# Block means of the values: from transposed sums on VectorE instead of twelve matmuls per head

## The chip, the core and the metric

One NeuronCore of a Trainium2 chip runs the whole program. Its engines each take their own instructions strictly in the order written: TensorE (PE) multiplies, VectorE (DVE) and ScalarE (ACT) work elementwise and reduce, GpSimd (POOL) does the same more slowly, and SyncE (SP) issues transfers between HBM and the core's memory. Engines meet through semaphores: an instruction may wait until a counter has reached a value, and everything behind it on its engine waits with it. The metric is the device time of one execution in microseconds.

## The reference

Attention with a window of 16 keys to either side of the query's own, plus one summary key and value per block of 32 keys, and behind it two layers of experts that this change leaves alone. With B = 4 batch elements, H = 8 heads, S = 768, D = 64:

```python
block, window = (32, 16)
nb = S // block                                     # 24
k_sum = k.reshape(B, H, nb, block, D).max(axis=3)
v_sum = v.reshape(B, H, nb, block, D).mean(axis=3)  # the block means of the values
scores_l = scale * np.matmul(q, k.transpose(0, 1, 3, 2))      # kept where |i - j| < window
scores_s = scale * np.einsum('bhsd,bhnd->bhsn', q, k_sum) + np.log(block)
a = softmax(concat([masked scores_l, scores_s]))
out = np.matmul(a, np.concatenate([v, v_sum], axis=2))
```

`v_sum` is what the change computes in another way.

## The kernel before

**Tiling.** The attention stage handles two heads at a time, a "pair": 4 batch elements of 4 pairs make 16 pairs, counted here by m = 0 to 15. A pair has PU = 3 units of 256 queries. A unit is: scores (L670, 16 matmuls, queries against a 96-key span and 24 block maxima), maxima on VectorE (L1231, L1234), exponentials on ScalarE (L998), a transpose (L679, copied out at L1006), the product with the values (L707, counted by the semaphore `pv_done`), the division on VectorE (L1240 to L1247, `x_done`), and a transpose of the result (L721).

**Steps.** All engines run the same software pipeline, written out by hand. In step n, TensorE does scores of unit n, the transpose of unit n-2, `values` of unit n-3 and `transpose_rows` of unit n-4. VectorE does `maxima` of unit n and `normalise` of unit n-3. ScalarE does the exponentials of unit n. `block_maxima` (the key summary) runs on VectorE in the steps with n % 3 of 0 and 1. Steps 0 to 5 are a prologue; a loop of 12 steps per batch element follows. The router's logits (L730, TensorE) and `route_shift` and `route` (VectorE) run in steps 14 to 17 of each group of 12, that is, in the steps 2 to 5 of the batch element that follows.

**Block means.** The values arrive as `va[m % 4]`, a tile with 96 keys on the partitions, for 12 overlapping windows of 64 queries, from the input `v_win` (585 KB per pair). `means` (L682 to L691) multiplies 12 slices of this tile by a constant matrix `average`, and accumulates them in a part of a PSUM bank, in step n = 3(m-1)+1 for pair m. `take_means` (L1198) copies the 24x128 result out in the same step, and GpSimd's `spread_means` (L528) writes it below the values, where L707 reads it. GpSimd builds `average` once at the start (L531 to L538).

**Transfers.** SyncE's queue loads keys and values. In its loop over batch elements, for each pair position hp (here G = 4b + hp, counted through), it waits for `spans_done` and issues the key load for the pair four later, then waits for `pv_done` of the last unit of pair G (reached in step 3G+5) and issues the value load for the pair four later. Since it is in order, the key load of position G is issued right behind the value load of position G-1. On the last batch element there is neither. At hp = 1 of a later batch element it also stores the last columns of `x` (L436). ScalarE's queue loads the queries (L980) in steps with n % 3 = 2 and stores `x` (L984) in steps with n % 3 = 0.

Of the kernel before, what the change touches and what calls it, by code (L numbers as in the profile page):

```python
# [10 lines left out]
ALU = mybir.AluOpType  # L11
ACT = mybir.ActivationFunctionType
AXX = mybir.AxisListType.X


P = 128
B, H, S, D = 4, 8, 768, 64
# [94 lines left out]

def two_layers_of_experts(nc, queries, k, v_win, modality_id, w_gate, modality_bias, w1, w2,
                          w_gate2, w1b, w2b, out):
    ctx = ExitStack()
    with ctx:
# [127 lines left out]
        k_loaded = [sem(f"k_loaded{i}") for i in range(HP)]  # L244
        vw_loaded = [sem(f"vw_loaded{i}") for i in range(HP)]
        pads_ready = sem("pads_ready")
        mask_ready = sem("mask_ready")
# [41 lines left out]
        span_mask = sa("span_mask", [P, PW])  # L289
        average = sa("average", [WK, NQ, NB])  # L290
        vst = [sa(f"vst{i}", [PW, 2, D]) for i in range(2)]
# [110 lines left out]
        def _(sp):  # L402
            def load_k(b, hp):
                sp.dma_start(kraw[hp][:, :, WINDOW:WINDOW + S], k[bass.ds(b, 1), hp, :, :, :].rearrange("o d h s -> (o d) h s")
                             ).then_inc(k_loaded[hp], 16)

            def load_v(b, hp):
                sp.dma_start(va[hp][0:WK, :, :, :], v_win[bass.ds(b, 1), hp, :, :, :, :].rearrange("o p h j w -> (o p) h j w")
                             ).then_inc(vw_loaded[hp], 16)

            load_k(0, 0)
            load_k(0, 1)
            load_v(0, 0)
            sp.dma_start(wg[:, :, :], w_gate.rearrange("(c p) e -> p c e", p=P)).then_inc(small_loaded, 16)
            sp.dma_start(bias2[:, :, :], bass.AP(modality_bias.tensor, 0, [[0, P], [E, 2], [1, E]])).then_inc(small_loaded, 16)
# [4 lines left out]
            with sp.Fori(0, B) as b:  # L420
                for hp in range(HP):
# [4 lines left out]
                    def refill_v(nb, nhp):  # L426
                        sp.wait_ge(pv_done, UNITS * b + PU * (hp + 1))
                        load_v(nb, nhp)

                    with sp.If(b < B - 1):  # L430
                        nb = nc.s_assert_within(b + 1, 0, B - 1, skip_runtime_bounds_check_because="b < B - 1 here")
                        refill_k(nb, hp)
                        refill_v(nb, hp)
# [54 lines left out]
        def _(pool):  # L488
# [35 lines left out]
            def spread_means(m):  # L524
                pool.wait_ge(means_taken, m + 1)
                if m >= HP:
# [3 lines left out]

            avg = average[:, :, :]  # L531
            pick = lambda pattern, base, per: chain(g.affine_select(out=avg, in_=avg, compare_op=ALU.is_ge, fill=0.0, base=base,
                                                                    pattern=pattern, channel_multiplier=per))
            chain(g.memset(avg, 1.0 / BLOCK))
            pick([[QB, NQ], [-BLOCK, NB]], -WINDOW, 1)
            pick([[-QB, NQ], [BLOCK, NB]], WINDOW + BLOCK - 1, -1)
            pick([[-2, NQ], [1, NB]], 0, 0)
            pick([[2, NQ], [-1, NB]], 1, 0)  # L538
            for t in va:
# [114 lines left out]
        def _(pe):  # L654
# [27 lines left out]
            def means(b, m, n):  # L682
                pe.wait_ge(vw_loaded[m % HP], 16 * (b + m // HP + 1))
                if m or not isinstance(b, int):
                    pe.wait_ge(means_taken, HP * b + m)
                if n >= 5:
                    pe.wait_ge(x_done, UNITS * b + n - 4)
                for j in range(NQ):
                    last = mm(bank[4 + (n + 1) % 2][WK:PW, MEAN0:MEAN0 + 2 * D], average[:, j, :], va[m % HP][0:WK, :, j, 0:D],  # L689
                              start=j == 0, stop=j == NQ - 1)  # L690
                last.then_inc(means_made, 1)  # L691

            def values(b, n):

                hp, i = n // PU, n % PU
                if i == 0:
                    pe.wait_ge(vsum_done, HP * b + hp + 1)
                pe.wait_ge(pt_out, UNITS * b + n + 1)
# [467 lines left out]
        def _(dve):  # L1166
# [12 lines left out]
            def block_maxima(b, m, h):  # L1179
# [6 lines left out]
                vec.tensor_reduce(ksum[:, h, :], own_keys, AXX, ALU.max).then_inc(bmax_done, 1)  # L1186

            def first_spans():
                dve.wait_ge(pads_ready, 1)
# [8 lines left out]
            def take_means(b, m, n):  # L1198
                dve.wait_ge(means_made, HP * b + m + 1)
                if n >= 3:  # L1200
                    dve.wait_ge(pv_done, UNITS * b + n - 2)
                if m >= 2:
                    dve.wait_ge(vsum_done, HP * b + m - 1)
                vec.tensor_copy(vst[m % 2][WK:PW, :, :].rearrange("p h d -> p (h d)"), bank[4 + (n + 1) % 2][WK:PW, MEAN0:MEAN0 + 2 * D]
                                ).then_inc(means_taken, 1)

            mask_rows(kbt[0])
            block_maxima(0, 0, 0)
            block_maxima(0, 0, 1)
            first_spans()  # L1210
            mask_rows(kbt[1])
            per = 10

# [37 lines left out]
            def unit(b, n, own):  # L1251
# [9 lines left out]
                if n % PU < 2:  # L1261
                    own(block_maxima, PU * m, m, n % PU)
                if n == 4:
                    token_biases()
# [454 lines left out]
def laid_out(inputs):  # L1719
# [10 lines left out]
    rows[..., :D] = _np.where(outside[:, :, None], 0, v[:, :, :, key, :]).transpose(0, 1, 4, 2, 3, 5)  # L1730
    laid["v_win"] = rows
    laid["moe2_w_gate"] = _np.asarray(inputs["moe2_w_gate"]).T
    return laid


_INS = ['q', 'k', 'v_win', 'moe_modality_id', 'moe_w_gate', 'moe_modality_bias', 'moe_w1', 'moe_w2',
        'moe2_w_gate', 'moe2_w1', 'moe2_w2']
# [19 lines left out]
```

## Time and profile before

| | us |
|---|---|
| median of 3 runs | 1066.01 (1064.84 to 1074.94) |
| the profiled execution | 1066.68, its span 1064.9 |
| attention stage | 0 to about 217 of the span |
| TensorE busy over the span | 898.2 (84%) |
| VectorE busy over the span | 681.6 (64%) |
| GpSimd busy over the span | 285.1 (27%) |
| `v_win` loads | 16 of 585 KB, median 6.4 us to landing |
| `k` loads | 16 of 384 KB, median 9.1 us to landing |

A granted clock of 1.00 stands for TensorE's 2.4 GHz, 0.50 for 1.2 GHz. The chain that ended last goes 27% through L777 and 11% through L898, which are the expert layers. Within the first 240 us it goes 17.0% through L689 (`means`), 14.0% through L670, 9.1% through L730, 8.9% through L707, 8.2% through L679.

### The profile page before, as it was taken

How to read it: one execution, taken by the hardware profiler on the slowest of the kernel's cores; microseconds unless marked ns; L12 is line 12 of the kernel's file. 1: busy time of each engine (PE TensorE's matmuls, PEld its weight loads, DVE VectorE, ACT ScalarE, POOL GpSimd, SP SyncE). 2: the span in 40 equal slices, each digit the busy share in tenths (PEclk: the TensorE clock that was granted, in tenths of full speed). 3: DMA queues.
4: the chain of work that ended last, by engine and by line, in shares of the span. 5: the costliest groups of instructions: out<-in, count | busy, mean ns of one | idle time of the engine just before them, and what ended most of it. 6: DMA issues, size and time to landing. Idle time of an engine off the chain costs nothing.

```text
span 1064.9 us, 21948 instructions
## 1 busy us (share of the span) xinstructions
PE 898.2 (84%) x7342; PEld 733.7 (69%) x7343; DVE 681.6 (64%) x1998; ACT 305.5 (29%) x626; POOL 285.1 (27%) x390
## 2 busy tenths in 40 slices
PE   4899999915899999999996233999898989998995
PEld 3787878714688888888885122868686867687884
DVE  5757576575666666666665567777777768674440
ACT  2544454505322212222221003223232322223330
POOL 5733344101012111111220005050515151414501
PEclk9999999956899999999998655999999999999998
DMA  9676675915011111111110123414141414155100
GB/s 195 122 160 135 133 153 100 280 50 185 11 51 40 50 40 40 40 40 40 40 50 20 24 71 119 159 51 169 50 169 54 165 61 159 61 204 172 32 29 30
DMA packets 45631, 99.94 MB, mean 94 GB/s; under 512 B 6736, under 2 KB 19072, under 8 KB 45440
## 3 DMA queue, kind: packets, MB, share of 16 engines
q1 hardware_dynamic: 26816, 61.63, 19.8%
q0 software_dynamic: 8064, 26.46, 7.9%
q10 hardware_dynamic: 10688, 11.01, 4.9%
q8 instruction: 39, 0.64, 0.2%
q14 instruction: 24, 0.20, 0.1%
HBM read 79.57 MB, written 19.51 MB: 93 GB/s over the span
## 4 chain that ended last, share of the span: by engine, by line
PE 69%; DVE 18%; issue 4%; POOL 3%; ACT 2%; DMA 2%; DVEq 0%; ACTq 0%; SPq 0%; POOLq 0%
PE bank L777 27%; PE bank L898 11%; PE bank L912 9%; PE bank L689 4%; PE bank L670 3%; PE bank L848 3%; DVE w_low L1649 2%; PE bank L730 2%; PE bank L707 2%; PE bank L801 2%; PE bank L679 2%; POOL slot_hot L635 2%; DVE xl L1653 1%; DVE ge L1517 1%; ACT xh L1042 1%
## 5 line engine op out<-in xcount | busy, mean ns | idle before, releaser
L1404 DVE SCALAR_TENSOR_TENSOR bank<-y,wg 128x512 f32<-128x512 f32 x200 | 132.0, 723 | 2.9
L635 POOL TENSOR_SCALAR slot_hot<-iota_l,mlo 128x128 bf16<-128x128 f32 x96 | 72.0, 766 | 214.7 <-DVE mlo L1622 214.7
L898 PE MATMUL bank<-xh,w_high 128*128 128x384 f32 x256 | 94.3, 368 | 16.1 <-DVE hl L1639 8.9
L777 PE MATMUL bank<-w_high,hh 128*128 x200 | 83.2, 416 | 13.2 <-DVE hl L1393 13.2
L777 PE MATMUL bank<-w_high,xh 128*128 x200 | 82.7, 414 | 10.7 <-DVE gates L1386 10.7
L592 POOL DMA_INDIRECT y_rows<-y,sidx x25 | 25.0, 998 | 243.2 <-DVE bank L1404 243.2
L898 PE MATMUL bank<-xh,w_low 128*128 128x384 f32 x256 | 88.1, 344 | 0.0
L898 PE MATMUL bank<-xl,w_high 128*128 128x384 f32 x256 | 87.9, 344 | 0.0
L1042 ACT ACTIVATE hh<-bank 128x512 fp32r<-128x512 f32 x50 | 27.1, 595 | 203.1 <-PE bank L801 203.1
L1418 DVE TENSOR_SCALAR y<-bank,gates 128x512 f32<-128x512 f32 x25 | 18.8, 751 | 101.1 <-PE bank L777 101.1
L912 PE MATMUL bank<-w_high,hh 128*128 128x512 f32 x192 | 82.3, 429 | 0.0
L1042 ACT ACTIVATE w_high<-w_landed 128x1024 fp32r<-128x1024 f32 x64 | 63.1, 1049 | 66.0 <-DMA w_landed<-in_moe_w 66.0
L777 PE MATMUL bank<-w_low,hh 128*128 x200 | 80.5, 403 | 0.0
L777 PE MATMUL bank<-w_high,hl 128*128 x200 | 80.3, 402 | 0.0
L777 PE MATMUL bank<-w_low,xh 128*128 x200 | 80.3, 402 | 0.0
L777 PE MATMUL bank<-w_high,xl 128*128 x200 | 80.2, 401 | 0.0
L1649 DVE TENSOR_TENSOR w_low<-w_landed,w_high 128x1024 fp32r<-128x1024 f32 x64 | 77.8, 1219 | 0.8
L848 PE MATMUL bank<-ge,cb 128*8 128x16 bf16 x1344 | 42.3, 170 | 41.7 <-DVE ge L1517 41.6
L912 PE MATMUL bank<-w_high,hl 128*128 128x512 f32 x192 | 75.7, 394 | 0.0
L912 PE MATMUL bank<-w_low,hh 128*128 128x512 f32 x192 | 75.5, 393 | 0.0
L848 PEld LDWEIGHTS bank<-ge,cb 128*8 128x8 bf16 x1344 | 36.2, 83 | 54.6 <-DVE ge L1517 50.8
L1118 ACT ACTIVATE hh<-bank 128x384 fp32r<-128x384 f32 x64 | 31.5, 492 | 140.2 <-PE bank L898 140.2
(285 smaller groups left out, 1932.5 us busy)
## 6 DMA issues: line engine op xcount, KB each, us to landing
w_landed<-in_moe_w SPq DMA_DIRECT2D x16, 2048.0 KB, 10.5
va<-in_v_win SPq DMA_DIRECT2D x16, 585.0 KB, 6.4
raw_w<-in_moe_w SPq DMA_DIRECT2D x4, 2048.0 KB, 11.3
k_raw<-in_k SPq DMA_DIRECT2D x16, 384.0 KB, 9.1
q_eye<-in_q ACTq DMA_DIRECT2D x16, 384.0 KB, 7.4
x_rows<-x ACTq DMA_DIRECT2D x12, 384.0 KB, 10.2
wg<-in_moe_w_gate SPq DMA_DIRECT2D x1, 2048.0 KB, 25.8
x_rows<-x SPq DMA_DIRECT2D x4, 387.0 KB, 7.2
```

The source lines that it names most:

```text
L592: pool.indirect_dma_start(out=dst[:, :], out_offset=bass.IndirectOffsetOnAxis(ap=sidx[:, 0:1], axis=0), in_=y[:, 0:w], in_offset=None).the ...
L635: last = g.tensor_scalar(slot_hot[:, j, :], iota_l[:, :], mlo[:, j:j + 1], None, ALU.is_equal)
L670: last = mm(bank[n % 2][QB * s_:QB * s_ + QB, PW * (2 * t + h):PW * (2 * t + h) + PW], qe[hp % 2][:, h, QB * j:QB * j + QB], kbt[hp % 2][: ...
L689: last = mm(bank[4 + (n + 1) % 2][WK:PW, MEAN0:MEAN0 + 2 * D], average[:, j, :], va[m % HP][0:WK, :, j, 0:D], start=j == 0, stop=j == NQ - 1)
L777: last = mm(ps, lhs[a][:, c, :], rhs[b](c), start=c == 0 and t == 0, stop=c == n - 1 and t == 2)
L848: last = mm(bank[7][0:E, 0:KSEARCH], cb[:, j, :], ge[:, j, :], start=j == 0, stop=j == TC - 1)
L898: last = mm(bank[fc % 2][:, 0:CAP], w[:, q % 2, c, f], a[:, c, :], start=c == 0 and t == 0, stop=c == KC - 1 and t == 2)
L912: last = mm(bank[2 + t % 2][:, :], a[:, c, rows], w[:, q % 2, c, :], start=c == 0 and n == 0, stop=c == FC - 1 and n == 2)
L1042: copy = lambda o, a: nc.scalar.activation(o, a, ACT.Copy)
L1118: nc.scalar.activation(hh2[:, fc, :], bank[fc % 2][:, 0:CAP], ACT.Relu).then_inc(hhigh_done, 1)
L1404: stt(bank[6 + e % 2][:, :], y[:, 0:DM], 1.0, wg2[:, e, :], ALU.mult, ALU.mult, accum_out=y[:, DM + e:DM + e + 1]).then_inc(l2_out, 1)
L1649: tt(low, whole, high.bitcast(F32), ALU.subtract).then_inc(low_done, 1)
```

## The change

The host lays out a second copy of the values, `v_cols`, of shape batch, pair, 2 x 64 head channels, 768 keys. SyncE loads 384 KB of it per pair into one of two new tiles `vcols`. VectorE sums 32 keys at a time (`sum_values`, a 128x768 reduction to 128x24, into one of two tiles `vsums`), for pair m in step 3m-4. TensorE turns this with one matmul against the identity in the step where `means` stood, and `take_means` multiplies by 1/32 as it copies. The constant `average` and its five GpSimd instructions are gone. The wait for the values' arrival moves from `means` to `values`.

```diff
@@ sync
+            def load_cols(b, m):
+                sp.dma_start(vcols[m % 2][:, :], v_cols[bass.ds(b, 1), m, :, :, :].rearrange("o h d s -> (o h d) s")
+                             ).then_inc(vc_loaded[m % 2], 16)
             load_k(0, 0)
             load_k(0, 1)
             load_v(0, 0)
+            load_cols(0, 0)
+            load_cols(0, 1)
...
+                    def refill_cols(cb_, m):
+                        sp.wait_ge(vsums_made, HP * b + m - 1)
+                        load_cols(cb_, m % HP)
+
+                    if hp < HP - 2:
+                        refill_cols(b, hp + 2)
                     with sp.If(b < B - 1):
                         nb = nc.s_assert_within(b + 1, 0, B - 1, skip_runtime_bounds_check_because="b < B - 1 here")
+                        if hp >= HP - 2:
+                            refill_cols(nb, hp + 2)
                         refill_k(nb, hp)
                         refill_v(nb, hp)
@@ gpsimd
-            avg = average[:, :, :]
...
-            chain(g.memset(avg, 1.0 / BLOCK))
@@ tensor
             def means(b, m, n):
-                pe.wait_ge(vw_loaded[m % HP], 16 * (b + m // HP + 1))
+                pe.wait_ge(vsums_made, HP * b + m + 1)
...
-                for j in range(NQ):
-                    last = mm(bank[4 + (n + 1) % 2][WK:PW, MEAN0:MEAN0 + 2 * D], average[:, j, :], va[m % HP][0:WK, :, j, 0:D],
-                              start=j == 0, stop=j == NQ - 1)
-                last.then_inc(means_made, 1)
+                mm(bank[4 + (n + 1) % 2][WK:PW, MEAN0:MEAN0 + 2 * D], vsums[m % 2][:, :], ident[:, :],
+                   start=True, stop=True).then_inc(means_made, 1)
@@ vector
+            def sum_values(b, m):
+
+                dve.wait_ge(vc_loaded[m % 2], 16 * (HP // 2 * b + m // 2 + 1))
+                if m >= 2:
+                    dve.wait_ge(means_made, HP * b + m - 1)
+                vec.tensor_reduce(vsums[m % 2][:, :], vcols[m % 2][:, :].rearrange("p (n t) -> p n t", t=BLOCK), AXX, ALU.add
+                                  ).then_inc(vsums_made, 1)
...
             first_spans()
+            sum_values(0, 0)
             mask_rows(kbt[1])
+            sum_values(0, 1)
...
                 if n % PU < 2:
                     own(block_maxima, PU * m, m, n % PU)
+                else:
+                    own(sum_values, PU * (m + 1), m + 1)
```

SyncE's queue, positions G = 0 and 1 of the first batch element, before. `k_raw` and `va` are the key and value tiles; the line of an ISA row is that of a wait.

```order
L404 ISA [waits spans_done]
L404 DMA k_raw0<-in_k 64x2x768
L427 ISA
L408 ISA [waits pv_done]
L408 DMA va0<-in_v_win 96x1560
L430 UNCONDITIONAL_BRANCH
L430 COMPARE_AND_BRANCH
L423 ISA
L404 ISA [waits spans_done]
L404 DMA k_raw1<-in_k 64x2x768
```

The same place now, from the value load of position 0 to that of position 1:

```order
L411 ISA [waits pv_done]
L411 DMA va0<-in_v_win 96x1560
L445 UNCONDITIONAL_BRANCH
L440 REGISTER_ALU
L415 ISA [waits vsums_made]
L415 DMA v_cols1<-in_v_cols 128x768
L445 COMPARE_AND_BRANCH
L407 ISA [waits spans_done]
L407 DMA k_raw1<-in_k 64x2x768
L436 ISA
L411 ISA [waits pv_done]
L411 DMA va1<-in_v_win 96x1560
```

The load of `v_cols` of position 1 (it is for pair 3) stands behind the wait for `pv_done` of position 0 and behind its value load, and ahead of the key load.

VectorE, the end of step 4 and step 5, before (`mbias` is the last of the token biases; then maxima of unit 5, division of unit 2, and the loop begins with step 6):

```order
L1223 TENSOR_TENSOR mbias<-mbias,mtmp 128x192 [waits dve_chain]
L1231 TENSOR_REDUCE nmax1<-bank1 128x4 [waits exp_done,scores_done,dve_chain]
L1234 TENSOR_SCALAR nmax1<-nmax1 128x4 [waits max_done]
L1240 TENSOR_SCALAR rtmp<-bank4 128x4 [waits pv_done]
L1242 RECIPROCAL rinv<-rtmp 128x4 [waits sums_read]
L1247 TENSOR_TENSOR x<-bank4,rinv 128x2x128 [waits inverted]
```

The same place now:

```order
L1241 TENSOR_TENSOR mbias<-mbias,mtmp 128x192 [waits dve_chain]
L1249 TENSOR_REDUCE nmax1<-bank1 128x4 [waits exp_done,scores_done,dve_chain]
L1252 TENSOR_SCALAR nmax1<-nmax1 128x4 [waits max_done]
L1258 TENSOR_SCALAR rtmp<-bank4 128x4 [waits pv_done]
L1260 RECIPROCAL rinv<-rtmp 128x4 [waits sums_read]
L1265 TENSOR_TENSOR x<-bank4,rinv 128x2x128 [waits inverted]
L1201 TENSOR_REDUCE v_sums1<-v_cols1 128x24 [waits means_made,vc_loaded1]
```

The sum of pair 3 stands at the end of step 5, ahead of all of step 6. The rows of the wait for `pv_done` are the same.

TensorE, step 7, before (scores of unit 7, transpose of unit 5, `means` of pair 3, `values` of unit 4):

```order
L670 MATMUL bank1<-k_bias0,q_eye0 64x120 x7
L679 MATMUL bank3<-ident,probs2 120x128 [waits pt_out,exp_done]
L679 MATMUL bank3<-ident,probs2 120x128 x3
L683 ISA
L689 MATMUL bank4<-va3,average 24x128 [waits x_done,means_taken,vw_loaded3]
L689 MATMUL bank4<-va3,average 24x128 x11
L707 MATMUL bank4<-va1,pt0 64x65 [waits x_done,pt_out]
```

And now:

```order
L679 MATMUL bank1<-k_bias0,q_eye0 64x120 x7
L688 MATMUL bank3<-ident,probs2 120x128 [waits pt_out,exp_done]
L688 MATMUL bank3<-ident,probs2 120x128 x3
L692 REGISTER_ALU
L697 MATMUL bank4<-ident,v_sums1 24x128 [waits x_done,means_taken,vsums_made]
L715 MATMUL bank4<-va1,pt0 64x65 [waits x_done,pt_out]
```

One matmul stands where 12 were (each f32 matmul shows twice in the trace), and it waits for VectorE's sum.

## Rows read from the trace of the kernel before

**Rows 1.** Windows of one pair and of one with logits: busy per engine, clock, DMA.

```profile
59.24:69.85 10.61, 10.43 (x139) 8.29 (x140) 7.09 (x19) 5.98 (x19) 4.78 (x7) 1.00 0.83 168
69.85:85.20 15.35, 15.35 (x187) 13.72 (x187) 8.41 (x21) 6.46 (x22) 6.17 (x8) 1.00 0.47 94
```

**Rows 2.** Groups by line and form, 0 to 240 us: count, busy us, mean ns, idle before.

```profile
L689 PE MATMUL bank<-va,average 96*24 96x128 f32 x384 | 47.4, 281 | 0.2 <-POOLq L541 0.2
...
L1186 DVE TENSOR_REDUCE ksum<-k_raw 64x24 f32<-64x768 f32 x32 | 29.8, 934 | 2.8 <-DMA k_raw<-in_k 2.8
...
L1204 DVE COPY vst<-bank 24x128 f32<-24x128 f32 x16 | 4.7, 297 | 36.0 <-PE bank L707 29.6 <-PE bank L689 6.3
```

**Rows 3.** Timeline 57 to 61 us, step 11 and the start of 12.

```profile
57.00 1.04 PE L670 MATMUL bank<-k_bias,q_eye 128*64 128x120 f32 x16
...
58.55 0.69 PE L707 MATMUL bank<-va,pt 120*64 120x65 f32 x16
...
58.74 0.64 DVE L1231 TENSOR_REDUCE nmax<-bank 128x4 f32<-128x480 f32 x1
...
59.43 0.33 SPq L408 DMA_DIRECT2D va<-in_v_win  x1
...
59.92 0.36 ACT L998 ACTIVATE probs<-bank,nmax 128x120 f32<-128x120 f32 x1
59.94 0.42 DVE L1247 TENSOR_TENSOR x<-bank,rinv 128x256 f32<-128x256 f32 x1
...
60.16 0.55 SPq L404 DMA_DIRECT2D k_raw<-in_k  x1
60.17 0.87 ACT L998 ACTIVATE probs<-bank,nmax 128x120 f32<-128x120 f32 x3
```

**Rows 4.** Timeline of SyncE's queue: first and last value load, and one with a store.

```profile
35.84 0.34 SPq L408 DMA_DIRECT2D va<-in_v_win  x1
...
96.15 0.33 SPq L408 DMA_DIRECT2D va<-in_v_win  x1
...
97.63 0.57 SPq L404 DMA_DIRECT2D k_raw<-in_k  x1
...
168.50 0.33 SPq L408 DMA_DIRECT2D va<-in_v_win  x1
```

**Rows 5.** Issues with us to landing: key loads at 36.6, 49.7 (158.6 alike), 86.2, 97.6, 148.7.

```profile
k_raw<-in_k SPq DMA_DIRECT2D x1, 384.0 KB, 6.3
...
k_raw<-in_k SPq DMA_DIRECT2D x1, 384.0 KB, 10.2
...
k_raw<-in_k SPq DMA_DIRECT2D x1, 384.0 KB, 5.8
...
k_raw<-in_k SPq DMA_DIRECT2D x1, 384.0 KB, 12.0
...
k_raw<-in_k SPq DMA_DIRECT2D x1, 384.0 KB, 9.4
```

**Rows 6.** The same for the first load behind the prologue's, issued at 12.3.

```profile
k_raw<-in_k SPq DMA_DIRECT2D x1, 384.0 KB, 15.6
```

**Rows 7.** Timeline of TensorE, 131 to 137 us: logits of unit 11, then step 17.

```profile
131.08 1.85 PE L730 MATMUL bank<-wg,xt 128*128 128x8 f32 x16
132.86 1.81 PE L670 MATMUL bank<-k_bias,q_eye 128*64 128x120 f32 x16
134.60 1.11 PE L679 MATMUL bank<-ident,probs 128*120 128x128 f32 x4
135.64 1.01 PE L707 MATMUL bank<-va,pt 120*64 120x65 f32 x16
```

**Rows 8.** Timeline of VectorE: the first and the last instruction of `route`, first batch element.

```profile
87.33 0.83 DVE L1278 TENSOR_TENSOR leq<-lg,lmax 128x48 f32<-128x48 f32 x1
...
90.53 0.17 DVE L1285 COPY x<-lidx 128x6 f32<-128x6 f32 x1
```

**Rows 9.** Windows again: step 17's end, and the weight prefetch after the attention's loads.

```profile
134.00:136.00 2.00, 2.00 (x18) 1.36 (x16) 1.97 (x3) 0.26 (x1) 1.76 (x2) 0.50 0.00 0
...
210.00:212.00 2.00, 2.00 (x18) 2.00 (x17) 0.00 (x0) 0.40 (x2) 0.00 (x0) 0.87 0.99 405
```

More of the change, by code:

```diff
@@ L110, in val, with two_layers_of_experts @@
     return k + x.c if x.c else k
-def two_layers_of_experts(nc, queries, k, v_win, modality_id, w_gate, modality_bias, w1, w2,
+def two_layers_of_experts(nc, queries, k, v_win, v_cols, modality_id, w_gate, modality_bias, w1, w2,
                           w_gate2, w1b, w2b, out):
@@ L245, in two_layers_of_experts @@
         vw_loaded = [sem(f"vw_loaded{i}") for i in range(HP)]
+        vc_loaded = [sem(f"vc_loaded{i}") for i in range(2)]
+        vsums_made = sem("vsums_made")
         pads_ready = sem("pads_ready")
@@ L289, in two_layers_of_experts @@
         span_mask = sa("span_mask", [P, PW])
-        average = sa("average", [WK, NQ, NB])
+        vcols = [sa(f"v_cols{i}", [P, S]) for i in range(2)]
+        vsums = [sa(f"v_sums{i}", [P, NB]) for i in range(2)]
         vst = [sa(f"vst{i}", [PW, 2, D]) for i in range(2)]
@@ L529, in spread_means @@
                 g.nop().then_inc(vsum_done, 1)
-            avg = average[:, :, :]
-            pick = lambda pattern, base, per: chain(g.affine_select(out=avg, in_=avg, compare_op=ALU.is_ge, fill=0.0, base=base,
-                                                                    pattern=pattern, channel_multiplier=per))
-            chain(g.memset(avg, 1.0 / BLOCK))
[L535 to L538, printed above, removed]
             for t in va:
@@ L696, in values @@
                 if i == 0:
+                    pe.wait_ge(vw_loaded[hp % HP], 16 * (b + hp // HP + 1))
                     pe.wait_ge(vsum_done, HP * b + hp + 1)
@@ L1203, in take_means @@
                     dve.wait_ge(vsum_done, HP * b + m - 1)
-                vec.tensor_copy(vst[m % 2][WK:PW, :, :].rearrange("p h d -> p (h d)"), bank[4 + (n + 1) % 2][WK:PW, MEAN0:MEAN0 + 2 * D]
-                                ).then_inc(means_taken, 1)
+                vec.tensor_scalar(vst[m % 2][WK:PW, :, :].rearrange("p h d -> p (h d)"), bank[4 + (n + 1) % 2][WK:PW, MEAN0:MEAN0 + 2 * D],
+                                  1.0 / BLOCK, None, ALU.mult).then_inc(means_taken, 1)
             mask_rows(kbt[0])
@@ L1731, in laid_out @@
     laid["v_win"] = rows
+    laid["v_cols"] = v.transpose(0, 1, 2, 4, 3)
     laid["moe2_w_gate"] = _np.asarray(inputs["moe2_w_gate"]).T
     return laid
-_INS = ['q', 'k', 'v_win', 'moe_modality_id', 'moe_w_gate', 'moe_modality_bias', 'moe_w1', 'moe_w2',
+_INS = ['q', 'k', 'v_win', 'v_cols', 'moe_modality_id', 'moe_w_gate', 'moe_modality_bias', 'moe_w1', 'moe_w2',
         'moe2_w_gate', 'moe2_w1', 'moe2_w2']
```

## The prediction

> **What bounds the kernel now.** I read three views. First the windows cut at SyncE's value loads, one pair of heads each [rows 1]: in a plain pair of 10.61 us TensorE is busy for 10.43, VectorE for 7.09, ScalarE for 5.98, GpSimd for 4.78. So TensorE sets the pace, and it also does where the logits come in (15.35 of 15.35). Then the groups by line [rows 2]: `means` is 47.4 us over 16 pairs, some 2.7 us of each pair, and about 5.3 in the first. What it is worth is at most that. Third the timeline of one step 11 with both queues in it [rows 3], because the change puts a new transfer into SyncE's queue and a new wait into VectorE's, and busy time says nothing of either.
>
> **What is saved.** 384 matmul records become 32. One matmul of two records is about 0.2 us, so TensorE loses 2.5 us per pair, 40 in all. GpSimd loses five short instructions at the start; they cost nothing, as VectorE will be waiting there for a transfer (below). The scaled copy in `take_means` is the same 24x128 copy of 0.30 us [rows 2].
>
> **What is added on VectorE.** Sixteen reductions of 128x768. The nearest row is the reduction of 64x768 with the same 768 elements on a partition, 0.93 us [rows 2]; I take it as it is. VectorE would be busy for 8.0 us of a pair, and TensorE for 7.9. Were there nothing else, a pair would take 8 to 9 us.
>
> **What is added as a wait, which decides.** The sum of pair m stands at the end of step 3m-4. Its transfer is issued by SyncE at position G = m-2, behind the wait for `pv_done` of position G-1. That is the `values` of unit 3G-1 = 3m-7, which TensorE executes in step 3G+2 = 3m-4. It is the same step, and VectorE's last work ahead of the sum (dividing unit 3m-7) waits for the same event. So the transfer is issued when VectorE is one division, under a microsecond, from needing it. The free buffer does not help: `vsums_made` was reached long before. SyncE is late because it is in order and waits for something else.
>
> Rows give the price. In step 11 `values` ends at 59.24 [rows 3]; call this V. SyncE issues the value load at V+0.2, and what stands next in its queue at V+0.9 (now keys, then `v_cols`, with keys behind it). VectorE has finished at V+1.1. The key load in that slot has the same 384 KB behind the same 585 KB, beside the same query load. Of the eleven such loads from 36.6 to 158.6, nine have no store of `x` on SyncE ahead of them; they land 5.8 to 10.2 us after issue, mean 8.3, the first 6.3 and the last 10.2 [rows 5]. I take 8.3. VectorE resumes at R = V+9.2.
>
> What is queued behind: on VectorE all of the next step, first the maxima, for which ScalarE's exponentials wait, then TensorE. TensorE still has step 3G+3 and the scores and transpose of 3G+4 to do, about 5 us, and then stops at the new matmul, which waits for the sum. This idle time is some 5 us per pair.
>
> From R to the next V: sum 0.93; maxima from R+1.0; the exponentials begin 1.18 after the maxima (58.74 to 59.92) and end 1.12 later (61.04) [rows 3], so R+3.3; the scores of step 3G+5, which wait for their bank, begin at R+3.5; from there to the end of `values` is 2.24 (57.00 to 59.24) [rows 3]. So V comes at R+5.8, and the period is 9.2 + 5.8 = 15.0 us instead of 10.6.
>
> **TensorE's clock.** Where it was granted 0.50, at 134 to 136 us [rows 9], the three groups on this path took 1.81, 1.11 and 1.01 us [rows 7] instead of 1.04, 0.65 and 0.69: the stretch of 2.24 becomes 3.8, and the transposes ahead of it add 0.3. A period is then 16.9. In this trace the attention stage kept 1.00 nearly throughout, but TensorE never idled 5 us in it, and the fall in [rows 9] came with no idle time, behind the logits' narrow matmuls. So the rows do not say what a stalled stretch gets, and both ends stand; I take the middle, 15.95.
>
> The Trainium skill, in "TensorE: Matmul & The Clock Gate", section "HAM oscillation — how this bites in real kernels", says that a wait for a transfer which repeats in every iteration sends the clock to half each time. By it the period would be 16.9 and the kernel some 1140 us. No row here shows it.
>
> **The sum.** Stalls come for pairs 3 to 14. (Pairs 0 and 1 are loaded at the start; on the last batch element SyncE no longer waits for `pv_done`, so pair 15 comes with pair 14.)
> - Start: pair 2's load goes into the slot of the key load issued at 12.3, which landed at 27.9 [rows 6]; with two more `v_cols` loads ahead, at some 2 us each, it lands at 32. The first V is at 37.8 instead of 35.6: +2.2.
> - Eleven periods, first to last value load, take 132.7 us now (35.84 to 168.50) [rows 4]. They become 11 x 15.95 = 175.5.
> - In two batch elements the logits of one unit, 1.7 us [rows 7], and `route`, 3.4 us from 87.33 to 90.70 [rows 8], lie between R and the next V: +10.2. The other logits and `route_shift` lie under the stall.
> - Twice a store of `x` stands ahead of the load: issued 1.48 instead of 0.73 behind the value load [rows 4], landing after 12.0 and 9.4 [rows 5] instead of 8.3: +6.3.
> - After the last stall TensorE has its earlier work done; the scores of step 41 come about 14.5 to 15 us behind V, where they now come 13.2 behind: +1.5. The last `means` saves 2.5: together -1.0.
>
> 2.2 + (175.5 + 10.2 + 6.3 - 132.7) - 1.0 = +60.5 us. Full clock throughout gives +50, half throughout +71 (with slower logits some +73). The profiled execution took 1066.7 and the median is 1066.0, so they are one number here: 1127 us, with 1116 and 1140 at the ends of the clock. With landings of 5.8 or 10.2 instead of 8.3 it would be 28 less or 21 more.
>
> **Rivals.**
> 1. *A stall at the full clock throughout*, 1116, or *at half throughout*, 1140. For the first speaks that this stage kept 1.00 through short gaps, for the second that the idle time is three or four times longer than any of them. 20% each.
> 2. *The transfer is quick.* The windows show 405 GB/s when large loads run alone [rows 9], against 168 in the attention stage [rows 1]. At 405, the 585 and 384 KB ahead and in it would take 2.4 us, and a landing of about 4 us would be possible. The eleven periods then cost 47 us less, and the kernel takes about 1080 or, at the full clock, 1069. Against it: the measured loads in this very slot. In "DMA: Bandwidth & Descriptors", section "Anatomy of one DMA — SWDGE (gpsimd) path", the Trainium skill gives 2.0 us plus the bytes at 436 GB/s, an estimate of 4.3 us for both together. The rows of this slot disagree with it by a factor of two, so I give the case 6%.
> 3. *The stall is hidden and the kernel faster.* The mechanism would be that the sum's load is in flight a step earlier, or VectorE a landing late anyway. The turning point is a landing of 3.8 us: 11 x (0.9 + 3.8 + 5.8) plus the other terms is 132.7. Fully hidden, VectorE at 8.0 us busy and TensorE at 7.9 give periods of about 9, and the kernel comes to 1066.7 - 11 x 1.6 - 5 for the slow first `means` - 5 for the last pairs = 1039. No row speaks for it; the order of SyncE's queue speaks against it. 3%.
> 4. *Contention*: the store of `x` by ScalarE now starts 2 to 3 us before the next burst rather than behind it, and takes engine time from the `v_cols` load; landings of 11 us give 1160. 8%.
>
> The forecast, a stall per pair with the clock between its levels, has 43%.
>
> **How the numbers follow.** Slower by over 1% (about what a measurement of this kernel tells from no change) holds forecast, 1, 4 and half of 2: 0.94. Within 1% is the rest of 2: 0.03. Faster is 0.03. The range drops rivals 2 and 3 and most of 4: from 1100 (full clock, landings of 6.8) to 1152 (half clock, landings of 9.3).
>
> **What would show it.** Right: VectorE idle ahead of the `v_cols` reduction with the transfer as releaser, some 8 us at a time, 12 times, about 95 in all; value loads of SyncE 15 to 17 us apart; the new matmul on TensorE waiting for VectorE; the attention stage ending near 277 instead of 217, and everything behind it unchanged. Wrong, if value loads stay below 11 us apart, if VectorE's wait is under 4 us, or if the stage's granted clock is 1.00 throughout (then 1116).

## The result, and the profile after

| | before | after |
|---|---|---|
| median, us | 1066.13 of 4 runs (1064.84 to 1074.94) | 1120.35 of 4 runs (1120.16 to 1120.9) |
| span of the profiled execution | 1064.9 | 1118.5 |
| last store of `x` by SyncE, the end of the attention stage | 217.70 | 267.37 |
| from there to the end of the span | 847.2 | 851.1 |
| first and last value load of SyncE's loop | 35.84, 168.50 | 36.96, 215.57 |

The ratio is 1.0477, 95% interval 1.044 to 1.0513: 54 us slower, where 61 were forecast. 49.7 of the 53.6 us between the spans lie in the attention stage. Ratios, here and below, go by executions in the chip's faster state alone; the profiled execution of `e2` was not in it, so only the ratio of `e2` is used.

The page of after, the busy times and the chain that ended last:

```profile
PE 893.5 (80%) x6990; PEld 722.9 (65%) x6991; DVE 683.6 (61%) x2014; ACT 305.6 (27%) x626; POOL 281.5 (25%) x385
...
PE 61%; DVE 17%; DMA 11%; issue 5%; ACT 2%; POOL 2%; SPq 1%; DVEq 0%; ACTq 0%; POOLq 0%
PE bank L785 25%; PE bank L906 11%; DMA v_cols<-in_v_cols 10%; PE bank L920 8%; PE bank L679 3%; PE bank L856 3%; DVE w_low L1669 2%; PE bank L738 2%; PE bank L715 2%; PE bank L809 2%; POOL slot_hot L644 2%; PE bank L688 1%; DVE xl L1673 1%; DVE ge L1537 1%; ACT xh L1050 1%
```

TensorE's busy time has hardly fallen (898.2 to 893.5), although 352 matmul records are gone. And the landing of `v_cols` is now a tenth of the chain. The waits, 0 to 290 us (engine, line, releaser: us in total, times, longest):

```profile
DVE v_sums L1201 <- DMA v_cols<-in_v_cols: 93.5, 15, 11.3
...
PE bank L697 <- DVE v_sums L1201: 50.6, 13, 8.4
```

The groups of the changed lines, which answer to [rows 2]:

```profile
L679 PE MATMUL bank<-k_bias,q_eye 128*64 128x120 f32 x768 | 63.3, 320 | 14.1 <-DVE k_bias L1212 10.8 <-POOLq L539 1.7 <-issue 1.3
...
L1201 DVE TENSOR_REDUCE v_sums<-v_cols 128x24 f32<-128x768 f32 x16 | 15.2, 952 | 93.5 <-DMA v_cols<-in_v_cols 93.5
...
L697 PE MATMUL bank<-ident,v_sums 128*24 128x128 f32 x32 | 8.1, 346 | 52.4 <-DVE v_sums L1201 50.6 <-DVE vst L1220 1.9
...
L1220 DVE TENSOR_SCALAR vst<-bank 24x128 f32<-24x128 f32 x16 | 4.8, 297 | 1.4 <-PE bank L715 0.7
```

47.4 us of `means` became 8.1. But the unchanged scores now take 320 ns a matmul. The kernel before took 279:

```profile
L670 PE MATMUL bank<-k_bias,q_eye 128*64 128x120 f32 x768 | 51.9, 279 | 18.8 <-DVE k_bias L1196 12.2 <-POOLq L522 4.2 <-DMA q_eye<-in_q 1.3
```

The timeline from the value load of position 1 to that of position 3, two periods (start, duration, engine, line, and in brackets the idle time before and its releaser):

```profile
51.57 0.34 SPq L415 DMA_DIRECT2D v_cols<-in_v_cols  x1
...
61.53 0.95 DVE L1201 TENSOR_REDUCE v_sums<-v_cols 128x24 f32<-128x768 f32 x1 [9.96 <-DMA v_cols<-in_v_cols]
...
62.53 0.62 PE L697 MATMUL bank<-ident,v_sums 128*24 128x128 f32 x2 [7.27 <-DVE v_sums L1201]
...
64.77 1.86 PE L679 MATMUL bank<-k_bias,q_eye 128*64 128x120 f32 x16
...
68.31 0.33 SPq L411 DMA_DIRECT2D va<-in_v_win  x1
...
69.01 0.35 SPq L415 DMA_DIRECT2D v_cols<-in_v_cols  x1
...
74.45 0.95 DVE L1201 TENSOR_REDUCE v_sums<-v_cols 128x24 f32<-128x768 f32 x1 [5.24 <-DMA v_cols<-in_v_cols]
...
81.36 0.33 SPq L411 DMA_DIRECT2D va<-in_v_win  x1
```

This is the loop of the prediction: issue, landing (9.9 and 5.4 us), VectorE stopped for it, TensorE stopped for VectorE, the path to the next value load, and with it the next issue. The windows show what each stop does to TensorE (us, busy of PE, PEld, DVE, ACT, POOL, clock, share of the transfer engines, GB/s):

```profile
56.00:60.00 4.00, 0.00 (x0) 0.00 (x0) 0.00 (x0) 0.00 (x0) 0.00 (x0) 1.00 1.03 212
60.00:64.00 4.00, 1.47 (x18) 1.07 (x18) 2.37 (x7) 0.72 (x3) 0.00 (x0) 0.55 0.30 63
64.00:68.00 4.00, 4.00 (x43) 3.05 (x40) 3.83 (x9) 2.84 (x9) 0.22 (x1) 0.60 0.37 102
68.00:72.00 4.00, 3.76 (x59) 2.91 (x56) 1.10 (x5) 2.51 (x8) 3.42 (x5) 1.00 0.66 175
...
40.00:160.00 120.00, 84.64 (x886) 66.67 (x887) 58.23 (x148) 44.63 (x137) 37.86 (x56) 0.76 0.64 140
```

For 4 us no engine works at all. When TensorE resumes, its clock is 0.55 and then 0.60 in two windows, and 1.00 in the third. The stall therefore costs twice: the idle time, and the slow stretch behind it, which stands on the path. How long that stretch lasts differs. Behind the stall that ended at 144.8 us logits followed, and the clock stood at 0.50 from 148 to 158 us, although TensorE was busy there without a break:

```profile
151.00:154.00 3.00, 3.00 (x16) 3.00 (x15) 0.70 (x3) 1.39 (x5) 2.70 (x3) 0.50 0.71 154
154.00:158.00 4.00, 4.00 (x34) 3.34 (x35) 0.00 (x0) 0.59 (x2) 1.32 (x2) 0.50 1.01 249
```

### The profile page after: what moved, and what is told of

The parts are those of the page before. It is cut to its first block, busy times and chain, and to the rows that moved or that the text cites. A ratio compares the mean times of both kernels' runs of the same rounds, so it can differ in the third digit from the quotient of the medians.

```text
span 1118.5 us, 21342 instructions
## 1 busy us (share of the span) xinstructions
PE 893.5 (80%) x6990; PEld 722.9 (65%) x6991; DVE 683.6 (61%) x2014; ACT 305.6 (27%) x626; POOL 281.5 (25%) x385
## 4 chain that ended last, share of the span: by engine, by line
PE 61%; DVE 17%; DMA 11%; issue 5%; ACT 2%; POOL 2%; SPq 1%; DVEq 0%; ACTq 0%; POOLq 0%
PE bank L785 25%; PE bank L906 11%; DMA v_cols<-in_v_cols 10%; PE bank L920 8%; PE bank L679 3%; PE bank L856 3%; DVE w_low L1669 2%; PE bank L738 2%; PE bank L715 2%; PE bank L809 2%; POOL slot_hot L644 2%; PE bank L688 1%; DVE xl L1673 1%; DVE ge L1537 1%; ACT xh L1050 1%
## 5 line engine op out<-in xcount | busy, mean ns | idle before, releaser
L785 PE MATMUL bank<-w_high,hh 128*128 x200 | 83.7, 419 | 15.0 <-DVE hl L1413 14.9
L906 PE MATMUL bank<-xh,w_low 128*128 128x384 f32 x256 | 88.2, 344 | 0.0
L1006 ACT ACTIVATE probs<-bank,nmax 128x120 f32<-128x120 f32 x192 | 53.4, 363 | 103.9 <-DVE nmax L1252 103.8
L679 PE MATMUL bank<-k_bias,q_eye 128*64 128x120 f32 x768 | 63.3, 320 | 14.1 <-DVE k_bias L1212 10.8
```

The lines of the kernel that those rows point to most:

```text
L679: last = mm(bank[n % 2][QB * s_:QB * s_ + QB, PW * (2 * t + h):PW * (2 * t + h) + PW], qe[hp % 2][:, h, QB * j:QB * j + QB], kbt[hp % 2][: ...
L785: last = mm(ps, lhs[a][:, c, :], rhs[b](c), start=c == 0 and t == 0, stop=c == n - 1 and t == 2)
L906: last = mm(bank[fc % 2][:, 0:CAP], w[:, q % 2, c, f], a[:, c, :], start=c == 0 and t == 0, stop=c == KC - 1 and t == 2)
L1006: last = nc.scalar.activation(probs[n % 3][:, a, :], bank[n % 2][:, PW * a:PW * a + PW], ACT.Exp, bias=nmax[n % 2][:, a:a + 1], scale=SCALE)
```

## The experiments

The median of before moved between the groups of runs (1066.8, 1072.2, 1069.1 and 1067.9 us), so ratios are compared. The other columns are each kernel's profiled execution: TensorE's granted clock and the busy share of the transfer engines in one window, and SyncE's last store of `x`.

| kernel | ratio to before, 95% | clock and share of transfer engines, 40 to 160 us | attention stage ends |
|---|---|---|---|
| before | 1 | 0.99, 0.73 | 217.7 |
| after | 1.0477 (1.044, 1.0513) | 0.76, 0.64 | 267.4 |
| `e1` after, load a pair earlier | 1.0005 (0.997, 1.0039) | 0.91, 0.89 | 215.3 |
| `e2` after, four buffers | 0.9964 (0.9923, 1.0004) | | |
| `e3` after, no `v_cols` reloads | 0.988 (0.9812, 0.9949) | 0.93, 0.80 | 207.3 |
| `e4` before, with the `v_cols` loads | 1.002 (0.9993, 1.0046) | 0.99, 0.91 | 216.6 |
| `e5` after, TensorE kept busy | 1.0457 (1.0365, 1.0549) | 0.94, 0.66 | 272.0 |
| `e6` after, sum a step later | 1.0454 (1.038, 1.0527) | 0.79, 0.66 | 262.3 |
| `e7` `e1` with four query buffers | 0.9972 (0.9939, 1.0004) | 0.91, 0.94 | 214.8 |
| `e8` before with four query buffers | 1.0007 (0.9976, 1.0038) | 0.99, 0.76 | 218.3 |
| `e11` `e1`, no key reloads | 0.9909 (0.9874, 0.9943) | 0.94, 0.78 | 205.6 |
| `e10` `e3`, no key reloads | 0.9735 (0.9682, 0.9787) | 0.96, 0.67 | 194.6 |
| `e12` before, change in even pairs | 0.9942 (0.9909, 0.9974) | 0.97, 0.84 | 213.7 |
| `e13` before, no key reloads | 1.0012 (0.9991, 1.0033) | 0.96, 0.53 | 220.5 |

What follows the attention stage took 846 to 855 us in these profiles, so a few microseconds of a total can come from there; the last column is free of that.

### Is it the place of the load, or its bytes?

`e1_pair_earlier`: the same loads, each one position earlier in SyncE's queue, and that of pair 2 ahead of the loop.

```diff
+            sp.wait_ge(vsums_made, 1)
+            load_cols(0, 2)
...
-                    if hp < HP - 2:
-                        refill_cols(b, hp + 2)
+                    if hp < HP - 3:
+                        refill_cols(b, hp + 3)
```

> The changed kernel, but SyncE issues the load of v_cols one pair earlier: at position G it loads pair G+3 and not G+2 (pair 2 goes ahead of the loop). Same loads, same two buffers, same waits on VectorE; only the place in SyncE's order moves. Theory (SyncE issues it in the step that needs it): a load now has a whole pair, 8 to 9 us, to land in some 7.7, so VectorE's wait falls from 93.5 us to under 15 and value loads of SyncE come 8.5 to 10 us apart; 1040 to 1055 us in all. Rival (the added traffic or VectorE's reductions cost it): the wait moves elsewhere and the time stays above 1090.

`e4_traffic`: the kernel before with the change's sixteen loads at the change's places, which nobody reads.

```diff
+                    def refill_cols(cb_, m):
+                        sp.wait_ge(vc_loaded[m % 2], 16 * (HP // 2 * b + m // 2))
+                        load_cols(cb_, m % HP)
```

> The kernel before, plus the 16 loads of v_cols at the very places in SyncE's queue where the change has them, which nobody reads; means stays with its 24 matmuls per pair. Theory: the traffic hides under TensorE, 1065 to 1075 (queries may land 1 to 2 us late in some pairs). Rival (contention of transfers is what costs the change its 54 us): above 1085.

Measured: 1068.03 us (ratio 1.0005) and 1069.24 (1.002). Moving the load alone takes all of the loss away, and the bytes alone cost nothing. So the place of the load in SyncE's order is the cause. But `e1` was expected at 1040 to 1055, and stayed level with before. The waits of `e1`, 0 to 240 us:

```profile
DVE v_sums L1203 <- DMA v_cols<-in_v_cols: 27.6, 8, 9.5
...
PE bank L681 <- DMA q_eye<-in_q: 12.5, 5, 6.3
```

VectorE's 93.5 us have shrunk to 27.6, and TensorE waits for queries, which it hardly did before. The same ten microseconds in `e1`, then in `e4`:

```profile
60.00:70.00 10.00, 4.96 (x42) 3.87 (x44) 2.64 (x7) 1.11 (x4) 3.10 (x5) 0.53 1.04 213
```

```profile
60.00:70.00 10.00, 10.00 (x131) 8.25 (x130) 6.99 (x18) 5.37 (x17) 4.17 (x7) 1.00 1.06 191
```

In both the transfer engines are full (share 1.04 and 1.06). In `e4` TensorE, with `means` still to do, is never stopped by them. In `e1` it has less to do, catches up with the loads, and stands. The timeline of `e1` shows for what:

```profile
65.05 1.87 PE L681 MATMUL bank<-k_bias,q_eye 128*64 128x120 f32 x16 [6.28 <-DMA q_eye<-in_q]
...
65.28 0.95 DVE L1203 TENSOR_REDUCE v_sums<-v_cols 128x24 f32<-128x768 f32 x1 [5.75 <-DMA v_cols<-in_v_cols]
```

Queries and `v_cols` are late together, and the scores behind the stop run at half clock (1.87 us instead of 1.04). The median landing of a query load between 40 and 160 us went from 7.5 us before to 11.0, that of a key load from 8.8 to 13.2.

The queries are issued by ScalarE and the added loads by SyncE. The Trainium skill, in "DMA: Bandwidth & Descriptors", section "Issuing engines are not separate DMA queues", says that loads of different issuers run on the same 16 engines and interleave. The trace agrees: with the added loads on SyncE's queue, the landings of ScalarE's query loads became longer too.

### More buffers

`e2_four_buffers`: four tiles for `v_cols`, loads four pairs ahead.

```diff
-        vc_loaded = [sem(f"vc_loaded{i}") for i in range(2)]
+        vc_loaded = [sem(f"vc_loaded{i}") for i in range(HP)]
...
-                        sp.wait_ge(vsums_made, HP * b + m - 1)
+                        sp.wait_ge(vsums_made, HP * b + m - 3)
...
-                        if hp >= HP - 2:
-                            refill_cols(nb, hp + 2)
+                        refill_cols(nb, hp + 4)
```

> The changed kernel with four v_cols buffers, each load issued four pairs ahead, as keys and values are; all four of the first batch element in the prologue, behind the keys and values of the same pair. Theory: no wait for v_cols in the loop at all; a pair is 8 to 9 us, set by VectorE (8.0 busy) and TensorE (7.9); 1035 to 1050, and no more than 8 us below the kernel that issues one pair earlier. Rival (transfers crowd each other): the stage is bound by landings of queries or keys, and it is no faster than the one-pair version.

`e7_four_queries`: `e1` with four tiles for the queries, loaded four pairs ahead. `e8_before_four_q`: the same tiles in the kernel before.

```diff
-                pe.wait_ge(q_loaded[hp % 2], 16 * (HP // 2 * b + hp // 2 + 1))
+                pe.wait_ge(q_loaded[hp % HP], 16 * (b + hp // HP + 1))
...
-                    m = n // PU + 2
+                    m = n // PU + HP
```

> The version that loads v_cols one pair earlier, and in addition four buffers for the queries instead of two, each loaded four pairs ahead. Theory (with the stall gone, the gain is eaten by queries that land late once pairs are shorter, and by the lower clock behind these waits): TensorE's wait for queries (12.5 us) is gone, pairs come 8.2 to 9.5 us apart, 1040 to 1052. Rival (VectorE, now as busy as TensorE, holds the pace by itself, or transfers as a whole): above 1060.

> The kernel before with the same four buffers for the queries, nothing else. Theory: queries were on time there in all but one place (1.3 us), so 1062 to 1067. Rival (late queries held the kernel before as well): under 1058.

Measured: 1065.92 (0.9964), 1068.8 (0.9972) and 1071.55 (1.0007). The first two miss what the theory of a single late load expected; for `e8` the ratio says, as expected, that queries did not hold the kernel before. In `e7` the wait for queries is gone, and the wait for `v_cols` stayed. The total between 30 and 210 us, and the longest of these waits:

```profile
DVE v_sums L1218 <- DMA v_cols<-in_v_cols: 30.1, 6, 12.8
...
36.41 0.95 DVE L1218 TENSOR_REDUCE v_sums<-v_cols 128x24 f32<-128x768 f32 x1 [12.83 <-DMA v_cols<-in_v_cols]
```

Median landings rose to 12.3 us (queries), 13.3 (`v_cols`), 14.5 (keys) and 11.5 (values, 6.0 before). Issuing earlier moved the wait from one load to another, and in `e7` 12.8 of its 30.1 us to the start, ahead of the sum of pair 2. With every landing longer, what is short is most likely transfer time. A version with four buffers for the queries and for `v_cols` together was not run.

### Taking bytes away

`e3_no_reload`: `v_cols` is loaded twice at the start, and never again. `e10_no_k_no_cols` leaves out the key loads behind the first batch element too. `e11_early_no_k` leaves these out in `e1`, and `e13_before_no_k` in the kernel before.

```diff
@@ e3
-                    if hp < HP - 2:
-                        refill_cols(b, hp + 2)
...
-                dve.wait_ge(vc_loaded[m % 2], 16 * (HP // 2 * b + m // 2 + 1))
+                dve.wait_ge(vc_loaded[m % 2], 16)
@@ e10, e11, e13
-                        refill_k(nb, hp)
...
-                    dve.wait_ge(k_loaded[m % HP], 16 * (b + m // HP + 1))
+                    dve.wait_ge(k_loaded[m % HP], 16)
```

> The changed kernel without any load of v_cols after the first two: every later pair sums the values of pair 0 or 1 again, so its block means are those of the wrong pair, and 14 loads of 384 KB are left out. It prices the change without its transfers. Theory: about 1030 to 1045, the saved matmuls minus VectorE becoming the bound; the difference to the four-buffer kernel is what the traffic costs, under 8 us. Rival (VectorE's 16 reductions are what costs): above 1060.

> The version that loads v_cols one pair earlier, without loading the keys again after the first batch element: later batch elements use the keys of the first, and 12 loads of 384 KB are left out. Theory (with v_cols the transfer engines are full at 175 to 190 GB/s and 10.6 us a pair, so TensorE's gain cannot show): with another 384 KB per pair gone, the volume is that of the kernel before, VectorE's wait for v_cols is under 10 us, and it takes 1050 to 1060, some 10 below the one-pair version. Rival (the engines' own order holds the pace): within 4 us of the one-pair version.

> The changed kernel without any load of v_cols after the first two and without loading the keys again: block means and keys of later pairs are those of earlier ones, 26 loads are left out. Theory (transfers set the pace): 1.39 MB a pair need about 8 us, as much as VectorE and TensorE; 1040 to 1050, 8 or more below the version that leaves out v_cols alone. Rival (below 1.8 MB a pair transfers no longer matter; VectorE and the chain from maxima to exponentials do): within 4 us of it.

> The kernel before without reloading the keys after the first batch element, so that the later ones use the first one's keys and the output is not the reference's. It is the control for the two kernels that gained 10 to 14 us from leaving the key loads out. Theory (in the kernel before TensorE sets the pace and the transfer engines have room, 0.81 of them busy between 40 and 80 us, so that bytes taken away buy nothing): 1065 to 1071, ratio 0.997 to 1.002. Rival (leaving the key loads out shortens any version by itself, because they delay the other loads or because VectorE or GpSimd start earlier): ratio 0.991 or less, some 10 us faster, and the gains of the other two kernels would say nothing of a second bound.

Measured: 1058.57 (0.988), 1061.38 (0.9909), 1044.88 (0.9735) and 1069.38 (1.0012). `e10` and `e13` lie in their expected ranges, `e11` 1 us above its own. `e3` missed its 1030 to 1045: without any wait for `v_cols` behind the start only 13 us were won, and its waits still show late queries:

```profile
PE bank L675 <- DMA q_eye<-in_q: 7.3, 4, 4.0
```

The four make one picture. In the changed kernel 384 KB less per pair are worth about 1% (`e11` against `e1`, `e3` against `e1`), and 768 KB less 2.7%. In the kernel before, the same key loads taken away are worth nothing (`e13`), nor do 384 KB more cost anything (`e4`). So in these kernels the bytes matter only where TensorE no longer covers them. The first two windows are of `e1` and `e10`, the last of `e13`:

```profile
40.00:80.00 40.00, 31.38 (x408) 24.54 (x408) 28.11 (x69) 20.22 (x62) 20.87 (x38) 0.87 0.97 187
```

```profile
40.00:80.00 40.00, 37.73 (x526) 30.13 (x526) 33.22 (x83) 24.42 (x76) 22.31 (x29) 1.00 0.72 138
```

```profile
40.00:80.00 40.00, 39.32 (x496) 32.39 (x497) 24.46 (x63) 21.20 (x65) 18.53 (x30) 1.00 0.57 122
```

`e1` holds the transfer engines at 0.97 and TensorE at 31.4 of 40 us. `e10`, with 0.72, has TensorE at 37.7 and does more of the kernel in the same time (VectorE 33.2 against 28.1). `e13` is TensorE's as before, at a share of 0.57.

### The clock, and the place of the sum

`e5_fill20`: twenty matmuls that nobody reads, ahead of the new matmul's wait.

```diff
+                if n >= 5:
+                    for _ in range(20):
+                        mm(bank[4 + (n + 1) % 2][:, 392:512], ident[:, :], ident[:, 0:120], start=True, stop=True)
+                pe.wait_ge(vsums_made, HP * b + m + 1)
```

> The changed kernel with 20 matmuls of 128x120 against the identity, in a part of the bank that nobody reads, ahead of each matmul that waits for VectorE's sum (pairs 3 on): some 4.5 us of work put into the idle time of the stall. Theory (the clock drops because TensorE idles in the stall, and costs about 0.9 us between VectorE's resumption and the next value load): the granted clock of the attention stage stays near 1.00, the scores behind the stall take 1.04 instead of 1.85 us, and the kernel takes 1108 to 1114 instead of 1120. Rival (the clock has nothing to do with it, or the filling is itself in the way): 1120 or more.

Measured: 1125.15 us, ratio 1.0457 (1.0365, 1.0549). Its timeline:

```profile
71.97 4.62 PE L698 MATMUL bank<-ident 128*128 128x120 f32 x40
...
75.69 0.95 DVE L1204 TENSOR_REDUCE v_sums<-v_cols 128x24 f32<-128x768 f32 x1 [7.25 <-DMA v_cols<-in_v_cols]
...
78.62 1.04 PE L679 MATMUL bank<-k_bias,q_eye 128*64 128x120 f32 x16
...
81.05 0.33 SPq L411 DMA_DIRECT2D va<-in_v_win  x1
```

The mechanism shows: the scores behind this stall take 1.04 us instead of 1.84 to 1.86, and from the sum to the value load it is 5.4 us instead of 6.8 and 6.9. The clock of 37 to 232 us rose from 0.80 to 0.93. Over all eleven periods the way from the start of the sum to the next value load took 80.8 us, in after 88.2, so in these two profiles the faster clock gave back some 7.5 us on the path. It could have been more: in seven of the twelve stalls the filling ended 0.7 to 3.3 us after the sum was ready, and held TensorE up.

The total does not show it: the expected 1108 to 1114 was not reached, and the interval includes both after's time and a gain of 12 us. In this profile the landings were longer (median of `v_cols` 7.8 us against 6.6 in after). From each value load to the start of the sum the eleven periods took 101.1 us instead of 90.4, which uses up the 7.5. Whether the filling lengthens the landings, or this one execution merely had longer ones, stays open, and with it what the clock is worth in the total.

`e6_step_later`: the sum moved from the end of a step to the next one, behind its maxima.

```diff
+                if n % PU == 0 and n:
+                    own(sum_values, PU * m, m)
...
-                else:
-                    own(sum_values, PU * (m + 1), m + 1)
```

> The changed kernel with VectorE's sum of pair m moved from the end of step 3m-4 into step 3m-3, behind the maxima of that step. The transfer and its place in SyncE's queue stay. Theory: VectorE waits for the same landing, but the maxima and ScalarE's exponentials of one more unit are done by then, so the way from its resumption to the next value load is 1.0 to 1.5 us shorter, 12 times: 1102 to 1110. Rival (what counts is the landing, and TensorE has its own wait for the sum): no more than 4 us below 1120.

Measured: 1117.83 us, ratio 1.0454 (1.038, 1.0527), not to be told from after; the expected 1102 to 1110 was missed. The waits, 0 to 290 us:

```profile
DVE v_sums L1201 <- DMA v_cols<-in_v_cols: 70.7, 14, 9.4
...
PE bank L697 <- DVE v_sums L1201: 57.7, 15, 7.9
```

VectorE waits 23 us less, TensorE 7 more, and the stage ends 5 us earlier. The consumer's place matters little while the load itself is issued this late.

### A version that takes part of the gain

`e12_even_pairs`: the change in every second pair only, so half the added bytes, and each load four pairs ahead.

```diff
+                        if hp % 2 == 0:
+                            sp.wait_ge(vsums_made, HP // 2 * b + hp // 2 + 1)
+                            load_cols(nb, hp)
...
+                if m % 2 == 0:
+                    mm(bank[4 + (n + 1) % 2][WK:PW, MEAN0:MEAN0 + 2 * D], vsums[m // 2 % 2][:, :], ident[:, :],
+                       start=True, stop=True).then_inc(means_made, 1)
+                    return
```

> The kernel before, with the change in even pairs alone (pairs 0, 2, 4...): they take their block means from v_cols by VectorE, loaded four pairs ahead with two buffers; odd pairs keep the 24 matmuls. Half the added traffic, half of TensorE's gain. Theory (transfers and TensorE share the pace): two pairs need 18.3 us of TensorE and 3.95 MB of transfers, 19.7 us at 200 GB/s, against 21.2 before: 1052 to 1062, the first version below the kernel before. Rival (transfers at 185 GB/s, 21.4 us for two pairs, hold it): 1064 or more.

Measured: 1065.88 us in 11 runs, ratio 0.9942 (0.9909, 0.9974): some 6 us faster than before, and faster than after by 5%. In absolute time that is 4 us above the upper end of its expectation, where the rival (1064 or more) had it; as a gain on before, whose median was 1069.1 here, it is near the lower end. It waits 7.8 us for queries where `e1` waits 12.5, and its clock of 40 to 160 us is 0.97: half the bytes, and nearly none of the stops.

## Why the prediction was right

**The wait.** Right, and it decides. The load is issued in the step that needs it; `e1` undoes only this and loses nothing any more. VectorE's idle time ahead of the reduction has the transfer as releaser, 12 times behind 35 us as forecast, 83.7 us in these (forecast about 95, some 8 at a time; measured 3.0 to 11.3, mean 7.0) and 93.5 with the three at the start. Value loads came 13 to 20 us apart, mean 16.2 (forecast 15 to 17), and the stage ended at 267.4 (forecast near 277).

**The size of the reduction.** 952 ns for 128x768 against 934 for 64x768 [rows 2]: right, and twice the partitions cost 2%.

**The path from sum to value load.** Forecast 5.8 us at full clock, 7.7 at half. Measured in the two periods above from the sum to the load's issue 6.8 and 6.9, less the 0.2 of the issue: the middle. Seven of the eleven periods took 6.3 to 7.3 us for it. The four with logits or `route` behind the sum took 9.4 to 11.0, together some 13 us more than plain ones, where 10.2 were forecast. The clock went as the forecast's middle had it, between the levels: low behind each stall of TensorE, 1.00 ahead of the next one, 0.76 over 40 to 160 us.

The prediction says that the trace before does not tell what a stalled stretch gets, as TensorE never idled 5 us in it. It had such a place at the start: behind 12.24 us of idle time the scores took 1.87 us instead of 1.04, though the clock column reads 1.00 there. That row spoke for a slow stretch behind the stall.

```profile
12.24 1.87 PE L670 MATMUL bank<-k_bias,q_eye 128*64 128x120 f32 x16 [12.24 <-DVE k_bias L1196]
```

The Trainium skill's section that the prediction cites ("TensorE: Matmul & The Clock Gate", "HAM oscillation — how this bites in real kernels") is borne out in kind: behind each of the eleven waits of TensorE for the sum the first scores took 1.78 to 1.87 us. Half clock throughout, as the prediction read it, would have given 1140 us; here the clock was back at 1.00 ahead of the next stall each time, and the time was 1120.

**The landing.** The term that was mis-sized. Forecast 8.3 us from the key loads of the slot. The nine `v_cols` loads of the first eleven without a store of `x` ahead landed after 5.4 to 9.9 us, mean 6.7. The two with a store took 10.5 and 9.8 (forecast 12.0 and 9.4). That is 9 x 1.6 + 1.1 = 15.5 us less than forecast. The price came from rows of a pipeline with all transfers close together; in the changed kernel they have longer periods to themselves (share 0.64 instead of 0.73). `e4` fits this: the same loads at the same places, with the periods of the kernel before, had median landings of 10.4 and 11.6 us (its two tiles).

Rival 2's price of 4.3 us is worked out from what the Trainium skill ("DMA: Bandwidth & Descriptors", "Anatomy of one DMA — SWDGE (gpsimd) path") fits to transfers issued by GpSimd. The loads here are SyncE's, and none of the eleven landed in less than 5.4 us from its own issue.

**The sum against the measurement**, in profiled spans:

| | forecast | measured |
|---|---|---|
| first value load later | 2.2 | 1.1 |
| eleven periods longer (all extras included) | 59.3 | 178.6 - 132.7 = 45.9 |
| from the last value load to the end of the stage | -1.0 | 51.8 - 49.2 = +2.6 |
| behind the attention stage | 0 | +3.9 |
| together | 60.5 | 53.6 |

The periods came 13.4 us short of the forecast, about the landings' 15.5; the logits made up part of this, as they run at half clock too when they follow a stall (3.42 us for those at 94.06 us, 1.85 for those at 81.37). The last two rows were not foreseen; the 3.9 is within what that part of the kernel varies between profiles. They lengthen the time, so the total is off by only 7 us where the periods are off by 13: that closeness is luck.

**The start.** Pair 2's sum began at 29.47 us, forecast 32: the two added loads cost less than assumed.

**A side claim that was wrong.** "Were there nothing else, a pair would take 8 to 9 us", and rival 3's 1039 for a hidden stall. The stall hidden (`e1`) gives 1.0005, not 0.974. The claim compared busy times of TensorE and VectorE, and left out the transfer engines as an engine. Per pair, values, keys, queries, `v_cols` and the store of `x` are 585 + 4 x 384 = 2121 KB (2.17 MB). In `e4` these moved at 175 GB/s with a share of 1.02, in `e1` at 187 with 0.97: an estimate from these rows is 11.6 to 12.4 us per pair. TensorE needed 10.6 for a plain pair, and 132.7 / 11 = 12.1 on average with the logits. So the added bytes brought the transfer engines' pace to about that of the kernel before, which fits all three versions that hide the stall (1.0005, 0.9964, 0.9972). Ratio 0.974 came only in `e10`, where 768 KB per pair are gone.

That the transfers set the pace of every period is argued and not shown. One profile each, in us:

| kernel | first value load | eleven periods | from the last value load to the end of the stage |
|---|---|---|---|
| before | 35.8 | 132.7 | 49.2 |
| `e1` | 40.2 | 126.6 | 48.5 |
| `e7` | 43.8 | 123.5 | 47.5 |
| `e3` | 33.8 | 123.0 | 50.6 |
| `e11` | 34.7 | 122.1 | 48.9 |

The average period was 11.5 us in `e1` and 11.2 in `e7`, below the estimate. `e7` with all its loads went through the eleven periods as fast as `e3` without them (which has two query buffers instead of four), and lost 8 us ahead of the first value load, where its longest wait stands. So a good part of what the added loads cost lies at the start, when the first loads land together. Neither this, nor the remaining clock loss in `e1` (0.91), nor its late loads were separated further: which share of its missing 27 us each has is open.

The chances: the landings and the clock were the two unknowns, and the time lies between rival 1's full clock (1116) and the forecast (1127), inside the range of 1100 to 1152. By the time alone rival 1 would be as near; the clock of 0.76 is what rules it out.

## What to carry to other kernels

Before adding a load to a queue that issues in order, write down which wait stands ahead of it and in which step that wait is met: here it was the step that needed the data, and moving the same load one position up was worth some 50 us (ratio 1.0477 to 1.0005). Before trading matmuls for bytes, count the transfer engines as an engine with a busy share of its own; in `e4` they were full beside a fully busy TensorE and cost nothing, and in `e1`, where TensorE has less to do, it stood waiting for them. A stall in front of TensorE also makes the work behind it slow, so price it as idle time plus a stretch at half clock.

## What the hardware showed that was not expected

The transfer engines were full (share 1.02) at 175 GB/s in `e4` with these loads and stores, where the weight loads reached 405 GB/s at 0.99 [rows 9]. The share alone therefore does not tell what rate is left.

One more load of 384 KB per pair lengthened every other one's landing, those of another issuer too (queries 7.5 to 10.0 us, keys 8.8 to 13.6, values 6.0 to 8.1 in `e4`), and the time did not change at all (1.002).

TensorE's clock was low behind every stall and back at 1.00 ahead of the next, but not after one fixed stretch: 0.55, 0.60 and 1.00 in the windows of 4 us above, and 0.50 from 148 to 158 us where logits followed. Eleven waits of TensorE for the sum, of 1.3 to 8.4 us, left 0.76 on average over 40 to 160 us, and not half.
